# Head-innermost q and v tiles, more dummy products at the start, and another order of the routed experts

## The reference

```python
# q, k, v: (4, 8, 576, 64); chunk 64, so 9 chunks
scores = scale * np.matmul(q_c, k_c.transpose(0, 1, 2, 4, 3))
attn = softmax(scores)                      # exp, sum + 1e-9
out = np.matmul(attn, v_c)
x = out.transpose(0, 2, 1, 3).reshape(2304, 512)

p = domain_probs / (domain_probs.sum(-1, keepdims=True) + 1e-09)
for e in range(4):                          # w1 (4,512,1024), w2 (4,1024,512)
    out += p[:, e:e+1] * (np.maximum(x @ w1[e], 0) @ w2[e])

logits = x @ w_gate                         # 8 experts
expert_idx = np.argmax(logits, axis=1)      # gate_w: its softmax probability
for e in range(8):
    out[mask] = gate_w[mask] * (np.maximum(xe @ w1[e], 0) @ w2[e])
```

## Time and profile before

| what | value |
|---|---|
| median of three runs | 1233.18 us (1231.43 to 1233.95) |
| the profiled execution, its own time | 1234.42 us |
| span of the profile, first to last instruction | 1232.6 us |
| TensorE products busy | 98% of the span |
| DVE, ACT, POOL busy | 38%, 22%, 26% |
| mean granted TensorE clock in the records | 0.994 |
| DMA | 81.11 MB, 92639 packets, 48255 of them under 512 B |

### The profile page before, as it was taken

One profiled execution on the slowest core, in us unless ns is written; L12 is line 12 of the kernel. 1 busy time (PEld: TensorE's weight loads), 2 busy tenths in 40 slices (PEclk: granted clock), 3 DMA queues, 4 the chain that ended last, 5 costly groups with the idle time before them and its releaser, 6 DMA issues.

```text
span 1232.6 us, 18555 instructions
## 1 busy us (share of the span) xinstructions
PE 1207.6 (98%) x6388; PEld 1070.5 (87%) x6389; DVE 462.6 (38%) x939; ACT 267.2 (22%) x416; POOL 315.5 (26%) x192
## 2 busy tenths in 40 slices
PE   8999999999999999999999999999998999999986
PEld 6999999999999999999999998899985888888875
DVE  4432442432222222222222223334356555555543
ACT  1222222223111113211112311122133011131420
POOL 7300000006000005100001500101047853185892
PEclk9999999999999999999999999999998999999998
DMA  9322112013000003000001200000273441272730
GB/s 245 78 52 55 47 51 60 9 49 97 1 0 0 0 0 119 17 0 0 0 0 59 77 26 27 1 25 26 79 181 118 123 149 72 68 249 73 252 129 21
DMA packets 92639, 81.11 MB, mean 66 GB/s; under 512 B 48255, under 2 KB 72959, under 8 KB 92610
## 3 DMA queue, kind: packets, MB, share of 16 engines
q1 hardware_dynamic: 84594, 67.88, 18.5%
q0 software_dynamic: 4416, 11.30, 3.0%
q10 hardware_dynamic: 3600, 1.57, 0.6%
HBM read 71.12 MB, written 10.92 MB: 67 GB/s over the span
## 4 chain that ended last, share of the span: by engine, by line
PE 91%; issue 2%; POOL 2%; DMA 2%; DVE 1%; ACT 1%; POOLq 0%; SPq 0%; DVEq 0%; ACTq 0%
PE psum L1135 14%; PE psum L1137 14%; PE psum L1136 14%; PE psum L1166 10%; PE psum L1168 10%; PE psum L1167 10%; PE psum L1338 3%; PE psum L1063 3%; PE psum L1340 3%; PE psum L1339 3%; PE psum L1080 3%; POOL weights_r L417 2%; PE psum L1325 1%; PE psum L1185 1%; DMA weights<-in_moe_w 1%
## 5 line engine op out<-in xcount | busy, mean ns | idle before, releaser
L417 POOL TENSOR_TENSOR weights_r<-weights,weights_r 128x1024 fp32r<-128x1024 f32 x96 | 232.1, 2443 | 678.6 <-ACT weights_r L570 677.8
L1135 PE MATMUL psum<-xhi,weights_r 128*128 128x384 f32 x768 | 261.0, 340 | 1.1 <-DVEq L724 0.4
L1137 PE MATMUL psum<-xhi,weights_r 128*128 128x384 f32 x768 | 257.0, 335 | 0.0
L1136 PE MATMUL psum<-xlo,weights_r 128*128 128x384 f32 x768 | 256.8, 334 | 0.0
L1166 PE MATMUL psum<-weights_r,hhi 128*128 128x512 f32 x576 | 228.7, 397 | 0.0
L1168 PE MATMUL psum<-weights_r,hlo 128*128 128x512 f32 x576 | 225.1, 391 | 0.0
L1167 PE MATMUL psum<-weights_r,hhi 128*128 128x512 f32 x576 | 224.5, 390 | 0.0
L730 DVE SCALAR_TENSOR_TENSOR hlo<-psum,hhi 128x384 fp32r<-128x384 f32 x192 | 106.9, 557 | 262.8 <-ACT hhi L565 262.8
L565 ACT ACTIVATE hhi<-psum 128x384 fp32r<-128x384 f32 x192 | 94.5, 492 | 510.8 <-PE psum L1137 510.3
L1135 PEld LDWEIGHTS psum<-xhi,weights_r 128*128 128x128 f32 x768 | 144.3, 188 | 4.3 <-DVE xlo L691 2.2
L1136 PEld LDWEIGHTS psum<-xlo,weights_r 128*128 128x128 f32 x768 | 144.3, 188 | 0.7
(11 more groups left out here) (172 smaller groups left out, 1147.8 us busy)
## 6 DMA issues: line engine op xcount, KB each, us to landing
weights<-in_moe_w SPq DMA_DIRECT2D x96, 512.0 KB, 5.4
qT<-in_q SPq DMA_DIRECT2D x36, 128.0 KB, 3.1
x_rows<-xfin SPq DMA_DIRECT2D x18, 256.0 KB, 2.3
kT<-in_k SPq DMA_DIRECT2D x15, 256.0 KB, 3.4
vbd<-in_v SPq DMA_DIRECT2D x30, 128.0 KB, 2.8
kT<-in_k ACTq DMA_DIRECT2D x3, 256.0 KB, 4.3
vbd<-in_v ACTq DMA_DIRECT2D x6, 128.0 KB, 7.3
meta<-slot_table SPq DMA_DIRECT2D x25, 1.0 KB, 2.5
```

What stands on the lines that cost most here:

```text
L417: gp.tensor_tensor(rounded(set_, 1, c), raw(set_, c), rounded(set_, 0, c).bitcast(F32), ALU.subtract).then_inc(sem("w_lo"), 1)
L1135: mm(out_, ahi, bhi, start=(i == 0), stop=False)
L1136: mm(out_, ahi, blo, start=False, stop=False)
L1137: last = mm(out_, alo, bhi, start=False, stop=(i == n - 1))
```

## The change

Three things change.

1. **Layouts.** q lies in HBM as `[B, NCH, DH, C, H]` instead of `[B, NCH, DH, H, C]`, and v has its head index last too. In SBUF `qT` becomes `[P, TG, P, H]` and `vbd` `[P, P, 2*KT]`. Each of the q and v loads moves the same 128 KB, now as one piece of 2 KB a partition instead of eight pieces of 256 B. The stationary operand of `score` and `attend` is `qT[:, j, :, h]` and `vbd[:, :, c*KT+r]`: its 128 columns lie 8 fp32 values (32 bytes) apart. k, and everything that is a moving operand, stays as it was.
2. **Dummy products.** Ten instead of nine at first; three instead of two inside each score block of the opening, after the second, fourth and sixth head; two more behind each of them. These are 10 more in all.
3. **The order of the experts.** Rank r gets the place min(2r, 15-2r). The places hold the ranks 0, 7, 1, 6, 2, 5, 3, 4. With the counts above, the experts 7, 6, 1, 0, 3, 5, 4, 2 stand there, with 6, 1, 6, 1, 4, 1, 2 and 2 blocks. The small chain of DVE instructions that works it out is one step shorter.

```diff
-    qT = tile("qT", [P, TG, H, P], F32, a0)
+    qT = tile("qT", [P, TG, P, H], F32, a0)
...
-    vbd = tile("vbd", [P, 2, KT, P], F32, a0 + 18432)
+    vbd = tile("vbd", [P, P, 2 * KT], F32, a0 + 18432)
...
             for j in range(TG):
                 for c in range(2):
-                    sp.dma_start(qT[c * DH:(c + 1) * DH, j, :, c * C:(c + 1) * C],
+                    sp.dma_start(qT[c * DH:(c + 1) * DH, j, c * C:(c + 1) * C, :],
                                  q_rows[j * P + c * DH:j * P + (c + 1) * DH]).then_inc(qk_in[j], 16)
...
-                vec.tensor_scalar(swap[:, :], rank_, -2.0, 16.0, ALU.mult, ALU.add)
-                then(vec.tensor_scalar(place_, rank_, 2.0, -1.0, ALU.mult, ALU.add), "order_step", 4)
+                vec.tensor_scalar(swap[:, :], rank_, -2.0, float(2 * E2 - 1), ALU.mult, ALU.add)
+                then(vec.tensor_scalar(place_, rank_, 2.0, None, ALU.mult), "order_step", 4)
+                vec.tensor_tensor(place_of[:, :], place_, swap[:, :], ALU.min)
                 then(vec.tensor_tensor(place_, place_, swap[:, :], ALU.min), "order_step", 5)
-                then(vec.tensor_scalar(place_of[:, :], place_, 0.0, None, ALU.max), "order_step", 6)
-                vec.tensor_scalar(place_, place_, 0.0, None, ALU.max)
...
                 for h in range(H):
-                    last = mm(psum[:, bank, h * C:(h + 1) * C], qT[:, j, h, :], kT[:, j, h, :], start=True, stop=True)
-                    if between is not None and h in (2, 5):
+                    last = mm(psum[:, bank, h * C:(h + 1) * C], qT[:, j, :, h], kT[:, j, h, :], start=True, stop=True)
+                    if between is not None and h in (1, 3, 5):
                         between(1)
...
-                        last = mm(psum[:, bank, r * P + c * C:r * P + (c + 1) * C], v_[:, c, r, :],
+                        last = mm(psum[:, bank, r * P + c * C:r * P + (c + 1) * C], v_[:, :, c * KT + r],
...
-            warm(9)
+            warm(10)
             pe.wait_ge(sem("q_zeroed"), 2)
             for j in range(TG):
                 pe.wait_ge(qk_in[j], 48)
                 score(j, j, Q0_B[j], warm)
+                warm(2)
```

More of the change, by code:

```diff
@@ L19, in chunked_attention_then_two_moes @@
     P = 128
-    B, NCH, DH, H, C = q.shape
+    B, NCH, DH, C, H = q.shape
     S = NCH * C
@@ L90, in chunked_attention_then_two_moes @@
     zrow = tile("zrow", [1, D], F32, at["xfin"] + 4096)
-    vbd0 = tile("vbd0", [P, 2 * TG, KT, P], F32, at["acc"])
+    vbd0 = tile("vbd0", [P, TG, P, 2 * KT], F32, at["acc"])
     probs0 = tile("probs0", [P, TG, H, C], F32, at["acc"] + 12288)
@@ L240, in source @@
         return a[:, :, r:r + RC, :].rearrange("o p r d -> (o p) r d")
-    q_rows = q.rearrange("b n d h s -> (b n d) h s")
+    q_rows = q.rearrange("b n d s h -> (b n d) s h")
     k_rows = k.rearrange("b n d h s -> (b n d) h s")
@@ L263, in load_v @@
                 for odd in range(2):
-                    sp.dma_start(vbd[odd * C:(odd + 1) * C, :, :, odd * DH:(odd + 1) * DH],
-                                 v[ds(t, 1), odd].rearrange("t s c r d -> (t s) c r d")).then_inc(v_in, 16)
+                    sp.dma_start(vbd[odd * C:(odd + 1) * C, odd * DH:(odd + 1) * DH, :],
+                                 v[ds(t, 1), odd].rearrange("t s d c r -> (t s) d (c r)")).then_inc(v_in, 16)
             def load_w(set_, m1, m2, e, c):
@@ L391, in _ @@
                              pattern=[[-1, P]], channel_multiplier=1).then_inc(sem("ident_ready"), 1)
-            gp.memset(qT[0:DH, :, :, C:2 * C], 0.0).then_inc(sem("q_zeroed"), 1)
-            gp.memset(vbd0[0:C, :, :, DH:2 * DH], 0.0).then_inc(sem("v0_zeroed"), 1)
-            gp.memset(vbd[0:C, :, :, DH:2 * DH], 0.0).then_inc(sem("v_zeroed"), 1)
+            gp.memset(qT[0:DH, :, C:2 * C, :], 0.0).then_inc(sem("q_zeroed"), 1)
+            gp.memset(vbd0[0:C, :, DH:2 * DH, :], 0.0).then_inc(sem("v0_zeroed"), 1)
+            gp.memset(vbd[0:C, DH:2 * DH, :], 0.0).then_inc(sem("v_zeroed"), 1)
             gp.memset(before[:, :], 1.0).then_inc(sem("c0"), 1)
@@ L548, in _ @@
                 for odd in range(2):
-                    act.dma_start(vbd0[odd * C:(odd + 1) * C, 2 * j:2 * j + 2, :, odd * DH:(odd + 1) * DH], v[j, odd])\
+                    act.dma_start(vbd0[odd * C:(odd + 1) * C, j, odd * DH:(odd + 1) * DH, :],
+                                  v[j, odd].rearrange("s d c r -> s d (c r)"))\
                         .then_inc(v_first[j], 16)
@@ L659, in spread @@
                 return a.unsqueeze(2).to_broadcast([a.shape[0], rows_, n])
-            vec.memset(qT[DH:2 * DH, :, :, 0:C], 0.0).then_inc(sem("q_zeroed"), 1)
-            vec.memset(vbd0[C:2 * C, :, :, 0:DH], 0.0).then_inc(sem("v0_zeroed"), 1)
-            vec.memset(vbd[C:2 * C, :, :, 0:DH], 0.0).then_inc(sem("v_zeroed"), 1)
+            vec.memset(qT[DH:2 * DH, :, 0:C, :], 0.0).then_inc(sem("q_zeroed"), 1)
+            vec.memset(vbd0[C:2 * C, :, 0:DH, :], 0.0).then_inc(sem("v0_zeroed"), 1)
+            vec.memset(vbd[C:2 * C, 0:DH, :], 0.0).then_inc(sem("v_zeroed"), 1)
             def shift(t, bank=Q_B, p=probs[:, :, :]):
@@ L839, in order_experts @@
                 then(vec.reduce_sum(rank_, cells, axis=X), "order_step", 3)
-                vec.tensor_scalar(swap[:, :], rank_, -2.0, 16.0, ALU.mult, ALU.add)
-                then(vec.tensor_scalar(place_, rank_, 2.0, -1.0, ALU.mult, ALU.add), "order_step", 4)
+                vec.tensor_scalar(swap[:, :], rank_, -2.0, float(2 * E2 - 1), ALU.mult, ALU.add)
+                then(vec.tensor_scalar(place_, rank_, 2.0, None, ALU.mult), "order_step", 4)
+                vec.tensor_tensor(place_of[:, :], place_, swap[:, :], ALU.min)
                 then(vec.tensor_tensor(place_, place_, swap[:, :], ALU.min), "order_step", 5)
-                then(vec.tensor_scalar(place_of[:, :], place_, 0.0, None, ALU.max), "order_step", 6)
-                vec.tensor_scalar(place_, place_, 0.0, None, ALU.max)
[L847 to L850, removed]
+                then(vec.tensor_scalar(swap[:, :], place_of[:, :], 2.0, float(8 * E2), ALU.is_ge, ALU.mult), "order_step", 6)
+                then(vec.tensor_tensor(cells, col(ids), row(place_), ALU.is_equal), "order_step", 7)
+                then(vec.tensor_tensor(cells, cells, row(ids), ALU.mult), "order_step", 8)
+                then(vec.reduce_sum(at_, cells, axis=X), "order_step", 9)
                 vec.tensor_copy(expert_at[:, :], at_).then_inc(sem("order_ready"), 1)
@@ L1073, in transpose_p, with attend @@
                 last.then_inc(sem("p_psum"), 1)
-            def attend(t, bank=K_B, v_=vbd[:, :, :, :], p_=pT[:, :, :], between=None):
+            def attend(t, bank=K_B, v_=vbd[:, :, :], p_=pT[:, :, :], between=None):
                 pe.wait_ge(sem("pT_ready"), t + 1)
@@ L1124, in _ @@
                 pe.wait_ge(v_first[j], 32)
-                attend(j, K0_B[j], vbd0[:, 2 * j:2 * j + 2, :, :], pT0[:, j, :, :], warm)
+                attend(j, K0_B[j], vbd0[:, j, :, :], pT0[:, j, :, :], warm)
             warm(5)
@@ L1407, in _laid_out @@
         b, h, s, d = a.shape
-        a = a.reshape(b, h, s // _CHUNK, _CHUNK, d).transpose(0, 2, 4, 1, 3)
+        a = a.reshape(b, h, s // _CHUNK, _CHUNK, d).transpose((0, 2, 4, 3, 1) if name == "q" else (0, 2, 4, 1, 3))
     if name == "v":
         b, h, s, d = a.shape
-        a = a.reshape(b, h // 2, 2, s // _CHUNK, _CHUNK, d).transpose(0, 3, 2, 4, 1, 5)
-        a = a.reshape(-1, 2, 2, _CHUNK, h // 2, d).transpose(0, 2, 3, 1, 4, 5)
+        a = a.reshape(b, h // 2, 2, s // _CHUNK, _CHUNK, d).transpose(0, 3, 2, 4, 5, 1)
+        a = a.reshape(-1, 2, 2, _CHUNK, d, h // 2).transpose(0, 2, 3, 4, 1, 5)
     return np.ascontiguousarray(a)
```

## The result

The changed kernel takes 1321.78 us (median of four, 1315.24 to 1329.03 us), the kernel before 1232.89 us in the same comparison. The ratio is 1.072, 95% interval 1.065 to 1.080. Forecast were 1223 us and a range of 1219 to 1253 us, so both the direction and the range were wrong. The profiled execution took 1329.03 us, its span is 1327.3 us.

The account below looks back on a forecast made before the run. TensorE's instruction stream, busy 98% of the span, was taken as the bound. From 1234.42 us, 6.2 us (opening) and 4.3 us (expert order) came off, giving 1223.9, stated as 1223 us; range 1219 to 1253 us.

Parts of the forecast that it names:

- The strided load: Score and attend weight loads: 32-byte steps on the stationary operand were taken to cost zero, so blocks stay at 1.75 us.
- the small DVE row: Vector-engine reads of 25 values, 183 ns at 32-byte steps against 173 ns for neighbours; at most 0.4 ns a value.
- the far bound: Score and attend loads: 576 loads, each 0.109 us longer, at the slowest pace any load shows; 63 us.
- The rule that I quoted: SBUF reads: 16-byte lines need at least two hits each; a new line for each access costs an unpriced penalty.
- The doubled load: Score and attend loads: rival in which each load takes twice as long, 63 us more, 1287 us; chance 0.13.
- The opening: Start to first hidden product: earlier q and an early clock rise bring hidden to 28.0 us, 6.2 us less.
- The q issues: Opening, SP queue: six issues of 0.8 us shrink to 0.4 us each, all done by 3.3 us instead of taking 4.83 us.
- the 5.8 us taken: Opening: q lands at 5.0 to 6.0 us and scores start at 5.8 us, 1.55 us earlier, with a 0.3 us gap.
- the clock stays low through the scores: Opening: rival with first transposes at 25.2 us, 3.1 us later, and 1233.2 us in all; chance 0.06.
- The order of the experts: Last expert, block 21: its first product no longer waits for POOL's rests of w1; 4.3 us less.
- q's wait: Opening: TensorE's 2.1 us wait for q was read as its second largest after the start.
- The main loop's traffic: Main loop: no wait for q or v shows, so the layout's larger pieces save nothing there.

Follow-up runs that it names:

- Experiment 6: Kernel before, packed layout kept, every score and attend product of the main loop issued twice; 1287.17 us, ratio 1.045.
- experiment 2: Kernel before with only the ten more dummies, layouts and expert order unchanged; 1231.22 us beside 1231.29 us, ratio 1.000.
- 8: Kernel before with the new expert order and 16 instead of 9 dummies at the start, layouts of before; 1225.33 us, ratio 0.9946.
- 9: Kernel before with new expert order, 16 starting dummies and the changed kernel's dummies in and behind the scores, layouts of before; 1225.05 us, ratio 0.9938.

## Why the prediction was wrong

**The strided load: the step that failed.** I bounded it by 0 and 63 us and took 0, with two reasons, and both were wrong. That a packed load runs at half the pace of the stream left a strided one no room: 128 columns went from 0.11 to 0.23 us, 0.9 ns more a column. And the small DVE row, 0.4 ns a value at most, said nothing about TensorE's port. In the blocks, the far bound was nearly right: 57 us in the loop, 1.9 us in the last attend, some 5.5 us in the three attends of the opening make 64 us against 63 us. Part of that agreement is luck: the bound counted the 48 loads of the opening's scores too, which cost almost nothing more at the low clock. The rule that I quoted from the Trainium skill (Advanced Engine Details and Errata, SBUF Cachelines) and set aside holds here: at a step of 8 bytes, two columns on a 16-byte line, a block costs 0.10 us more, and at 16 bytes, one column on a line, the load takes twice as long. I had given that rival 0.13. Its evidence deserved more: nothing in the trace of before showed a strided load on that engine, and the loads were what set the pace.

**The clock: not in any rival.** The doubled load was priced at 1287 us and came out at 1322 us. Of the difference, 28 us lie in the loop, where some 63 us of dense products ran at 1.2 GHz behind strided blocks. The trace of before had shown the clock low through 12 us of score passes in the opening; I used it for the dummies and did not ask it of the 30 blocks that the same change would thin out. Experiment 6 has blocks of the same length and no such loss.

**The opening.** The sum had 6.2 us less; the trace has 9.9 us more up to the first score block of the loop, of which 5.5 us are the strided attends. The q issues did not shrink to 0.4 us; the six took 3.77 us instead of 4.83 us, 0.59 us each. The mean of 0.8 us in the forecast was that of a median of 0.63 us and one issue of 1.43 us. q landed at 6.8 us instead of the 5.8 us taken, so a gap of 1.1 us was left. The clock did not rise in the scores. This was the rival "the clock stays low through the scores": it gave the first transposes at 25.2 us, and they came at 24.92 us. That they agree so closely is in part luck: the scores started 1.0 us later than it had them, and their blocks and the dummies behind them were shorter. That denser dummies or a row up to the scores can bring the clock up early is real (experiments 2, 8 and 9). But the changed kernel stayed low with a gap of 1.1 us, where experiment 2, with the same dummies and packed loads, rose behind one of 1.7 us. So the open gap alone does not explain it; whether the strided loads of its scores or chance made the difference stays open, with one trace of each.

**The order of the experts: right.** Forecast 4.3 us, 3.9 us measured alone, and the wait is gone in the changed kernel's trace too. No other load came late. The forecast's reading that q's wait was the second largest of TensorE was wrong: two waits for DVE, 2.6 us and 2.2 us in all, stood ahead of it. Nothing in the sum rests on them.

**The main loop's traffic: right.** 32,000 packets less and no time for them: no wait for q or v was there to go.

## What to carry to other kernels

Where a product has fewer columns than its stationary operand, the weight load is the pace, and an edit that makes a load strided should be priced at the doubled load until a run says otherwise. A step of 8 bytes between fp32 columns cost 0.1 us a block here. The stride on the 64 moving columns beside a packed load cost as little; what it costs where the moving side is the pace was not measured. A layout for larger DMA pieces is worth its trouble only where a transfer is waited for. And a strided stretch can cost again in the dense work behind it: read the granted clock there too, and count the low time in dense work alone.

## What the runs showed that I had not expected

- The cost of the step is a cliff: score blocks of 1.76, 1.86, 3.70 and 3.78 us at 4, 8, 16 and 32 bytes.
- At the low clock, strided passes cost little more than packed ones: 0.80 us for four in the changed kernel's opening (8.23 to 9.03 us) against 0.75 us in experiment 2. In the loop a strided block takes 3.78 us at a granted clock of 0.50 and of 0.82.
- On the moving side the 32-byte step costs 0.08 us a block where on the stationary side it costs 2.0 us.
- The changed kernel's four runs are 14 us apart (1315.24 to 1329.03 us), where four of the kernel before are 2.5 us apart. The two shorter ones have a mean granted clock of 0.958 and 0.960, the two longer ones 0.953 and 0.947. The clock falls some twenty times in the loop; where its steps fall seems to matter, but this was not tested.
